# Hash products of a masked-attention kernel in three 32-column strips of the array, with their loads reordered

## What is computed

```python
# q, k, v: batch 2, heads 8, sequence 768, head width 64; proj: 64 x 6
q_bits = einsum('bhsd,dk->bhsk', q, proj) > 0        # six bits for each query
k_bits = einsum('bhsd,dk->bhsk', k, proj) > 0        # and for each key
mask = (q_bits as a number) == (k_bits as a number)
scores = where(mask, q @ k.T / sqrt(64), -1e9)
attn = softmax(scores) @ v                            # x = attn, heads side by side
g = s * relu(x @ w_in) ** 2 + b;  x = g @ w_out       # feed-forward, s and b scalars
e = argmax(x @ w_gate + bias[modality])               # routing to one of eight experts
out = softmax gate * relu(x @ w1[e]) @ w2[e]
```

## Time and profile before

| | us |
|---|---|
| median of three runs | 732.97 |
| their range | 732.0 to 734.8 |
| profiled execution, its own time | 731.03 |
| its span in the trace | 729.2 |
| TensorE busy | 704.5 (97%) |
| VectorE busy | 428.0 (59%) |
| ScalarE busy | 321.6 (44%) |
| GpSimd busy | 266.8 (37%) |

### The profile page before, as it was taken

The page is one execution under the profiler, slowest core; times in us unless marked ns, Lnnn a source line. Parts: engine busy times, 40 slices in busy tenths (PEclk is TensorE's granted clock), DMA queues, the critical chain, the costliest instruction groups (busy, mean ns, idle before and its releaser), DMA issues.

```text
span 729.2 us, 12070 instructions
## 1 busy us (share of the span) xinstructions
PE 704.5 (97%) x3810; PEld 587.8 (81%) x3810; DVE 428.0 (59%) x825; ACT 321.6 (44%) x634; POOL 266.8 (37%) x271
## 2 busy tenths in 40 slices
PE   7799999999999999999999999999999899999994
PEld 3389999999999987888888888888885688877883
DVE  0589999999999956548555643564197611333110
ACT  0078878788787854221222221123144223443221
POOL 0666777677667751007004500720001222121111
PEclk9989999999999999999999999999999999999999
DMA  9921321321233030001100300001135541001011
GB/s 296 264 59 55 105 55 55 97 65 54 80 81 117 1 116 0 1 2 58 58 1 0 115 0 0 1 8 51 58 132 183 190 161 59 29 30 45 32 56 47
DMA packets 22508, 51.32 MB, mean 70 GB/s; under 512 B 3168, under 2 KB 5344, under 8 KB 22464
## 3 DMA queue, kind: packets, MB, share of 16 engines
q1 hardware_dynamic: 19008, 42.34, 18.3%
q0 software_dynamic: 2480, 7.87, 3.3%
q10 hardware_dynamic: 976, 0.56, 0.3%
HBM read 44.47 MB, written 6.55 MB: 70 GB/s over the span
## 4 chain that ended last, share of the span: by engine, by line
PE 89%; DVE 4%; DMA 2%; ACT 1%; issue 1%; SPq 1%; ACTq 0%; POOL 0%; POOLq 0%; DVEq 0%
PE ps L1373 9%; PE ps L1392 9%; PE ps L1576 6%; PE ps L1578 6%; PE ps L1577 6%; PE ps L1540 6%; PE ps L1542 6%; PE ps L1541 6%; PE ps L1406 5%; PE ps L1407 5%; PE ps L1661 3%; PE ps L1663 3%; PE ps L1662 3%; PE ps L1631 3%; PE ps L1633 3%; PE ps L1632 3%
## 5 line engine op out<-in xcount | busy, mean ns | idle before, releaser
L678 ACT ACTIVATE pt_hi<-ps 128x384 fp32r<-128x384 f32 x192 | 88.0, 499 | 42.1 <-PE ps L1392 26.9
L939 DVE TENSOR_TENSOR pt_lo<-ps,pt_hi 128x384 fp32r<-128x384 f32 x192 | 100.1, 551 | 10.4 <-ACT pt_hi L678 6.3
L731 ACT ACTIVATE relu<-ps 128x512 f32<-128x512 f32 x48 | 28.7, 598 | 175.6 <-PE ps L1542 175.6
L667 ACT ACTIVATE probs<-ps,neg_max 128x768 f32<-128x768 f32 x96 | 87.3, 909 | 26.0 <-DVE neg_max L930 25.9
L1392 PE MATMUL ps<-cst,probs 128*128 128x128 f32 x576 | 90.7, 275 | 0.9 <-DVE pt_lo L939 0.9
L930 DVE TENSOR_REDUCE neg_max<-ps 128x1 f32<-128x768 f32 x96 | 90.9, 946 | 0.0
L1117 DVE TENSOR_TENSOR sq<-relu 128x512 f32<-128x512 f32 x48 | 36.4, 759 | 71.6 <-ACT relu L731 71.2
L1540 PE MATMUL ps<-xt_hi,wi_hi 128*128 128x512 f32 x192 | 75.8, 395 | 0.0
L1576 PE MATMUL ps<-wo_hi,g_hi 128*128 128x512 f32 x192 | 74.9, 390 | 0.6 <-DVE xt_lo L1007 0.6
L1392 PEld LDWEIGHTS ps<-cst,probs 128*128 128x128 f32 x576 | 70.6, 145 | 5.9 <-DVE pt_lo L939 1.6
L1542 PE MATMUL ps<-xt_hi,wi_lo 128*128 128x512 f32 x192 | 74.8, 390 | 0.0
(11 more groups left out here) (198 smaller groups left out, 1473.0 us busy)
## 6 DMA issues: line engine op xcount, KB each, us to landing
w_raw<-w SPq DMA_DIRECT2D x16, 512.0 KB, 6.8
raw_k<-kT SPq DMA_DIRECT2D x32, 192.0 KB, 3.3
raw_q<-qT SPq DMA_DIRECT2D x32, 192.0 KB, 3.6
wi_raw<-w_in SPq DMA_DIRECT2D x4, 1024.0 KB, 5.1
wo_raw<-w_out SPq DMA_DIRECT2D x4, 1024.0 KB, 5.1
pair_raw<-qT SPq DMA_DIRECT2D x8, 384.0 KB, 6.7
pair_raw<-kT SPq DMA_DIRECT2D x8, 384.0 KB, 13.6
raw_v<-v SPq DMA_DIRECT2D x16, 192.0 KB, 2.4
```

Source lines behind the costliest of these rows:

```text
L939: nc.vector.tensor_tensor(pt_lo[c % 2][sl], unit(tt, h).rearrange("p (k q) -> p k q", k=3), pt_hi[c % 2][sl].bitcast(F32), ALU.subtract).t ...
```

## The change

- The 96 columns are cut into three strips of 32 (`STRIPS`): strip 0 has pairs 0, 1, 2; strip 1 has 2, 3, 4, 5; strip 2 has 5, 6, 7. Pairs 2 and 5 lie across a border and are multiplied in two strips. Each product has a stationary operand of 128x32 and writes 32 PSUM rows. There are ten (pair, strip) tasks for a side where eight products stood, in four rounds (`ROUNDS`); within a round the tasks alternate between strips, first all in 512 columns and then all in 256.
- `first_masks(0)` stands before the third round of the k side, which is after four tasks.
- q and k pairs are loaded in the order 2, 5, 0, 3, 6, 1, 4, 7 (`ARRIVAL`).
- For the first pair only one half of `raw_k[z]` and `raw_q[z]` is loaded, two loads of 64 partitions for a head where there were four (`load_half`). The other half of `ka` and `qa` is made from `pair_raw`, pair 0 (`split_first`): seven GpSimd operations in place of six. The head loads of head 0 stand after k pairs 2, 5, 0.
- Of the constants only `patt` and `cst` are loaded early. ScalarE waits for the last k pair and then issues the other five, on a semaphore `late_in` that TensorE, ScalarE and VectorE wait for after the attention.
- In the loop over the later pairs only the counts of `qk_split` are shifted by two.

```diff
-PAIRS_BEFORE_HEAD = 2
+STRIP = 32
+STRIPS = ((0, 1, 2), (2, 3, 4, 5), (5, 6, 7))
+ROUNDS = (((2, 0), (5, 2), (2, 1)), ((5, 1),), ((0, 0), (3, 1), (6, 2)), ((1, 0), (4, 1), (7, 2)))
+ARRIVAL = (2, 5, 0, 3, 6, 1, 4, 7)
...
-            for n in range(PIECES):
+            for n in ARRIVAL:
                 load_pairs(0, n)
+            def load_half(z):
+                n = half(z, False)
+                for dst, src in ((raw_k[z], kT), (raw_q[z], qT)):
+                    sp.dma_start(dst[n, :], src[z, :, :]).then_inc(raw_in[z], 16)
...
-            for n in range(PAIRS_BEFORE_HEAD):
+            for n in ARRIVAL[0:3]:
                 load_pairs(1, n)
-            load_head(0, 0, True)
-            for n in range(PAIRS_BEFORE_HEAD, PIECES):
+            load_half(0)
+            for n in ARRIVAL[3:]:
                 load_pairs(1, n)
             load_v(0, 0, True)
-            load_head(0, 1, True)
+            load_half(1)
             load_v(0, 1, True)
...
+            def split_first(z):
+                m, n = half(z, True), half(z, False)
+                done = 7 * z
+                pool.wait_ge(pairs_in[PIECES], 16)
+                copied(ka[z][m, :], pair_raw[m, 1, 0, :], 1.0, qk_split, done + 1)
+                copied(qa[z][m, :], pair_raw[m, 0, 0, :], SCALE, qk_split, done + 2)
+                pool.wait_ge(raw_in[z], 32)
+                copied(ka[z][n, :], raw_k[z][n, :], 1.0, qk_split, done + 3)
+                rest_qk(z, n, done + 1)
...
-            act.wait_ge(pairs_in[0], 16)
-            for dst, src in ((cst[:, :], consts), (patt[:, :], patterns), (tri_sb[:, :], tri), (sb_sb[:, :], sb_rows),
-                             (wg_sb[:, :, :], w_gate), (mid_sb[:, :, :], mod_id), (mb_sb[:, :, :], mod_bias)):
+            act.wait_ge(pairs_in[ARRIVAL[0]], 16)
+            for dst, src in ((patt[:, :], patterns), (cst[:, :], consts)):
                 act.dma_start(dst, src).then_inc(const_in, 16)
+            act.wait_ge(pairs_in[PIECES + ARRIVAL[-1]], 16)
+            for dst, src in ((tri_sb[:, :], tri), (sb_sb[:, :], sb_rows), (wg_sb[:, :, :], w_gate),
+                             (mid_sb[:, :, :], mod_id), (mb_sb[:, :, :], mod_bias)):
+                act.dma_start(dst, src).then_inc(late_in, 16)
...
             for c in range(2):
-                for j in range(PAIRS):
-                    if j % PIECE == 0:
-                        pe.wait_ge(pairs_in[PIECES * c + j // PIECE], 16)
-                    if c == 1 and j == 2:
+                for n, tasks in enumerate(ROUNDS):
+                    if c == 1 and n == 2:
                         first_masks(0)
                     for lo, hi in ((0, 512), (512, SEQ)):
-                        last_mm = mm(banks[0:NH * NBITS, 1024 * c + lo:1024 * c + hi], projb[:, j, :],
-                                     pair_raw[:, c, j, lo:hi], start=(j == 0), stop=(j == PAIRS - 1))
+                        for j, t in tasks:
+                            pe.wait_ge(pairs_in[PIECES * c + j], 16)
+                            strip = slice(STRIP * t, STRIP * t + STRIP)
+                            last_mm = mm(banks[strip, 1024 * c + lo:1024 * c + hi], projb[:, j, strip],
+                                         pair_raw[:, c, j, lo:hi], start=(n == 0), stop=(n == len(ROUNDS) - 1))
                 last_mm.then_inc(proj_done, 1)
             first_masks(1)
```

More of the change, by code:

```diff
@@ L292, in program @@
         const_in = sem("const_in")
+        late_in = sem("late_in")
         projb_in = sem("projb_in")
@@ L407, in _, with load_head @@
             sp.dma_start(projb[:, :, :], proj_blocks).then_inc(projb_in, 16)
-            for n in range(PIECES):
+            for n in ARRIVAL:
                 load_pairs(0, n)
-            def load_head(i, z, first):
-                if not first:
-                    sp.wait_ge(qk_split, i * 12 + (6 * z - 6))
+            def load_half(z):
+                n = half(z, False)
+                for dst, src in ((raw_k[z], kT), (raw_q[z], qT)):
+                    sp.dma_start(dst[n, :], src[z, :, :]).then_inc(raw_in[z], 16)
+            def load_head(i, z):
+                sp.wait_ge(qk_split, i * 12 + (6 * z - 4))
                 for dst, src in ((raw_k[z], kT), (raw_q[z], qT)):
@@ L426, in load_v, with load_heads @@
                     "a p t d -> (a p) t d")).then_inc(v_in[z], 16)
-            def load_heads(i, first):
+            def load_heads(i):
                 for z in range(2):
-                    load_head(i, z, first)
-                    load_v(i, z, first)
-            for n in range(PAIRS_BEFORE_HEAD):
+                    load_head(i, z)
+                    load_v(i, z, False)
+            for n in ARRIVAL[0:3]:
                 load_pairs(1, n)
-            load_head(0, 0, True)
-            for n in range(PAIRS_BEFORE_HEAD, PIECES):
+            load_half(0)
+            for n in ARRIVAL[3:]:
                 load_pairs(1, n)
             load_v(0, 0, True)
-            load_head(0, 1, True)
+            load_half(1)
             load_v(0, 1, True)
             with sp.Fori(1, PAIRS) as i:
-                load_heads(i, False)
+                load_heads(i)
             def load_quarter(q, first):
@@ L521, in copied, with split_qk, rest_qk @@
                 pool.wait_ge(signal, count)
[L523 to L528, removed]
+            def split_qk(i, z):
+                pool.wait_ge(raw_in[z], i * 64 + 32)
+                pool.wait_ge(scores_done, i * TILES_PER_PAIR + (QT * (z + 1) - TILES_PER_PAIR))
                 m, n = half(z, True), half(z, False)
-                done = i * 12 + 6 * z
+                done = i * 12 + (6 * z + 2)
                 copied(ka[z][:, :], raw_k[z][:, :], 1.0, qk_split, done + 1)
                 copied(qa[z][m, :], raw_q[z][m, :], SCALE, qk_split, done + 2)
+                rest_qk(z, n, done)
+            def split_first(z):
[7 more added lines that the diff above has]
+                rest_qk(z, n, done + 1)
+            def rest_qk(z, n, done):
                 copied(qb[z][n, :], raw_q[z][n, :], SCALE, qk_split, done + 3)
@@ L564, in pair @@
             def pair(i):
-                split_qk(i, 0, False)
+                split_qk(i, 0)
                 place_masks(i, 0)
@@ L568, in pair @@
                 place_masks(i, 1)
-                split_qk(i, 1, False)
+                split_qk(i, 1)
                 split_v(i, 1, False)
             for z in range(2):
-                split_qk(0, z, True)
+                split_first(z)
                 split_v(0, z, True)
@@ L772, in keep_exp @@
                                      ACT.Exp).then_inc(lexp_done, 1)
+            act.wait_ge(late_in, 16 * 5)
             quarter(0, True, False)
@@ L894, in _ @@
         def _(v_):
-            v_.wait_ge(const_in, 16 * 7)
+            v_.wait_ge(const_in, 16 * 2)
             nc.vector.memset(row_sum[:, :, :, 1], 1e-9).then_inc(eps_known, 1)
@@ L1156, in _ @@
             quarter(0, True, False)
+            v_.wait_ge(late_in, 16 * 5)
             then(V.tensor_copy(midf[:, :], mid_sb[:, :, 0]))
@@ L1328, in first_masks @@
                 if c == 0:
-                    pe.wait_ge(const_in, 16 * 7)
+                    pe.wait_ge(const_in, 16 * 2)
                 else:
@@ L1366, in scores @@
                 if j == 0:
-                    pe.wait_ge(qk_split, i * 12 + (6 * z + 6))
+                    if first:
+                        pe.wait_ge(qk_split, 7 * z + 7)
+                    else:
+                        pe.wait_ge(qk_split, i * 12 + (6 * z + 8))
                     pe.wait_ge(masks_in, i * 4 + (2 * z + 2))
@@ L1583, in quarter @@
                                 early_list()
+            pe.wait_ge(late_in, 16 * 5)
             quarter(0, True, False)
```

## The result

| | before | changed |
|---|---|---|
| median of 20 executions, us | 732.13 | 727.28 |
| their range, us | 730.04 to 737.56 | 725.18 to 731.8 |
| span of the profiled execution, us | 729.2 | 724.0 |
| mean granted clock in it | 0.994 | 0.998 |
| first score product, us | 33.26 | 29.35 |

What follows compares the result with a forecast made beforehand. The prediction took the start's loads, ending with the last k pair at 24.0 us, as the bound. First scores 5.4 us earlier, less 0.4 for the clock, gave 5.0: 732.97 - 5.0 = 728.0 us, range 724.8 to 733.5.

Steps and rivals of the forecast that it cites:

- Strips overlap, by halves: Hash products: two records on different strips run at once, so a task costs 0.64 us instead of 1.28 alone.
- Fully: strip 1 has four tasks: Hash products, bound with full overlap: the strip with four tasks sets a side's time, 5.1 us.
- Weight loads stay hidden: Hash products: loads of 0.16 us stay under running records; if they waited for a neighbour's matmul, up to 12.8 us more.
- The loads decide: Start, k side: the last k pair's landing at 24.0 us sets the side's end at 25.3 and first scores at 27.9.
- so I run the queue at 385 GB/s from 15 us on: Load queue at the start: with small constants moved last, 385 GB/s holds from 15 us, without the 240 GB/s stretch.
- The slow stretch: Load queue before the change: 240 GB/s, placed where the five small constants and their short rows are in flight.
- about 0.5 MB more than its own place: Landing rule at the start: a load lands when about 0.5 MB beyond the bytes issued up to and with it has moved.
- 2.56 us from the last product to the scores: From the k side's last hash product to the first score product: path unchanged, 2.56 us as before.
- The clock: First scores: the drop to half clock comes a little earlier, both first tiles run at 1.2 GHz, 0.4 us dearer.
- The rival of a starved k side at 1.2 GHz: K side waiting for loads loses the full clock: 729.5 to 732.5 us, chance 22% of the clock rival's 30%.
- The sum: Whole kernel: first scores 5.4 us earlier, less 0.4 for the clock, 5.0 us gained, giving 728.0 us.
- Cover on the other engines: Start: GpSimd ends 1.2 us before TensorE asks, head 1 is covered by 2.8 us, ScalarE's table load by 1.9.

Runs made afterwards that it cites:

- the kernel with fewer bytes: Changed kernel with 0.66 MB less loaded ahead of the last k pair (packed projection blocks, only parts of `cst` and `patt` early): median 726.27 us, ratio to before 0.9909.

## Why the prediction was right or wrong, point by point

- **Strips overlap, by halves: wrong, they overlap in full, and the sum did not feel it.** The prediction took two records in flight and 0.64 us a task. The clearest rows are the k side's first two rounds in the kernel with fewer bytes:

```profile
4.39 10.72 PE L1378 MATMUL ps<-pair_raw,projb 128*32 128x512 f32 x42 [4.39 <-DMA pair_raw<-qT]
...
15.46 2.77 PE L1378 MATMUL ps<-pair_raw,projb 128*32 128x512 f32 x14 [0.35 <-DMA pair_raw<-kT]
```

  The first row holds the 40 records of the q side and two of the k side, the 512 columns of its first task. The second holds the other 14 of these two rounds: six of 512 columns and eight of 256, alone 6 x 0.43 + 8 x 0.21 = 4.3 us. Narrow windows of the timeline, from 15.46 to 15.48 and from 16.52 to 16.55, show how they start:

```profile
15.46 0.62 PE L1378 MATMUL ps<-pair_raw,projb 128*32 128x512 f32 x3 [0.35 <-DMA pair_raw<-kT]
...
16.34 0.39 PE L1378 MATMUL ps<-pair_raw,projb 128*32 128x256 f32 x2
```

  Three records, by the order of the tasks one on each strip, are in flight at once, and up to 16.34 us the 512, 512 and 256 columns of three strips ran side by side: 2.1 us of work in 0.88. The whole 2.77 is what strip 1 needs for its own columns in these rounds, 0.86 + 0.43 + 1.28 = 2.57, and 0.2 until its last record ends. This is the prediction's other bound, "Fully: strip 1 has four tasks". The factor of 2.4 agrees with the 2.38x of the Trainium skill ("TensorE: Matmul & The Clock Gate", Part 3) for three column tiles. For the sum it made no difference, because the loads decided: behind the last pair stood 1.49 us where 1.3 were forecast, and that is the last strip's own 512 and 256 columns, 1.28, and the same 0.2.
- **Weight loads stay hidden: right.** The 80 loads of 32 columns took 0.11 us each as the middle value, and ran while TensorE had no gap from 13.53 for 5.73 us. The rule of the Trainium skill ("TensorE: Matmul & The Clock Gate", Part 3), that loads overlap only matmuls of other row groups, is not what these rows show.
- **The loads decide: right in kind, 1.3 to 2.3 us too early.** "It lands at 24.0": it landed at 25.3 and 26.3. The failing step is "so I run the queue at 385 GB/s from 15 us on": from 15 us to the landing it ran at 322 GB/s in the first trace and at 301 in the second. The slow stretch was put down to small constants alone. They are one cause, as the runs with early constants show, but loads into 64 partitions are the other, and two of those stay ahead of the last pair. This is a mis-sized term in the right sum. The rule "about 0.5 MB more than its own place" came from one landing: in twelve traces the surplus was 0.4 to 0.8 MB, a spread that is worth a microsecond.
- **2.56 us from the last product to the scores: right** (29.35 - 26.80 = 2.55).
- **The clock: wrong in sign.** The prediction took 0.4 us for an earlier fall. In the profiled execution there was none, worth 1.2 us, and over all executions the change has the higher clock, worth 1.0, which is weakly shown. The rival of a starved k side at 1.2 GHz did not occur in either trace of the change. What in the new order favours the clock was not isolated.
- **The sum** came right (5.0 against 4.9) by luck, because the two errors cancel: 3.9 instead of 5.4 at the first scores, and 1.0 to 1.2 gained by the clock instead of 0.4 lost.
- **Cover on the other engines: right**, with smaller margins for head 1 (1.45 us instead of 2.8) and larger ones for the table load (2.7 instead of 1.9).
- **What carried the gain.** The prediction said less on this than it should: it priced the whole, and not strips and loads apart. Either alone gives part of it by the executions (2.6 us each at equal clock), since products and loads were two bounds of nearly the same length.

## What to carry to other kernels

Where a stage has products and loads of nearly the same length, a cheaper product gains only up to the next landing, so count the bytes ahead of the last load that it needs, and price them at the rate of their form. Move what is not needed yet behind it: small rows above all, then columns of constants that no one reads until later. Before a difference of a microsecond is explained by an edit, compare the granted clock of the executions, and take a second trace.

## What the runs showed of the hardware

- float32 matmuls of 128x32 on three different column strips ran side by side, and those of one strip one after the other: work that takes 2.1 us alone took 0.88 us on three strips, and two rounds took as long as the strip with the most columns.
- Loads into 64 partitions moved at about 199 GB/s with a full queue, loads into 128 at 400. Run beside full loads they left no stretch near 200 GB/s in that time. In one pair of kernels the last landing came no earlier by it and in another it did, so the price of that form is not settled, and no run shows what limits it.
- Five constants of 0.10 MB in short rows delayed the last pair by 1.9 to 3.6 us in two traces, and cost 1.5 us of time at equal clock.
- One kernel's mean granted clock ranged from 0.984 to 0.998 between executions, and its time by some 7 us with it. The traces show falls to half speed of some 4 to 8 us each. Seven lie at the first scores (29 to 42 us), one at the k side (22 to 27) and one from 551 to 558 us, where TensorE's records leave no gap; which of them comes differed from one execution to the next. A wait of 2.05 us for the third k pair was followed by a fall in one trace, and one of 2.69 us at the same place in another trace was not.
